# Routing of the first three batches spread over the attention heads, and the first expert's weights split inside the last heads

## What is computed

```python
q_n, k_n = rmsnorm(q, g_q), rmsnorm(k, g_k)
attn = softmax(q_n @ k_n.T / 8);  x = attn @ v          # 48 heads of 448 x 64
logits = (x / |x|) @ (emb / |emb|).T / tau               # x as 1792 rows of 768
expert = argmax(logits);  gate = softmax(logits)[expert]
y = gate * (relu(x @ w1[expert]) @ w2[expert])           # w1 768x1024, w2 1024x768
h = y @ w_in;  out = max(0.01 * h, h) @ w_out            # 768 -> 2048 -> 768
```

## Time and profile before

| | |
|---|---|
| time of the profiled execution, span | 1319.03 us, 1317.3 us |
| median of 3 runs | 1318.18 us |
| PE busy | 1237.8 us, 94% |
| DVE busy | 891.9 us, 68% |
| ACT busy | 748.0 us, 57% |
| POOL busy | 558.2 us, 42% |
| mean granted TensorE clock, share of full | 0.972 |
| attention / experts / feed-forward, about | 0 to 378, 378 to 802, 802 to 1317 us |

### The profile page before, as it was taken

One profiled execution on the slowest core, in us unless ns is written; L12 is line 12 of the kernel. 1 busy time (PEld: TensorE's weight loads), 2 busy tenths in 40 slices (PEclk: granted clock), 3 DMA queues, 4 the chain that ended last, 5 costly groups with the idle time before them and its releaser, 6 DMA issues. The chain is left out here.

```text
span 1317.3 us, 21043 instructions
## 1 busy us (share of the span) xinstructions
PE 1237.8 (94%) x6906; PEld 1101.8 (84%) x6906; DVE 891.9 (68%) x1267; ACT 748.0 (57%) x1420; POOL 558.2 (42%) x638
## 2 busy tenths in 40 slices
PE   5999999997878899999999986999999999999998
PEld 4888888876767789888999975899999999999997
DVE  4889999997574899999999993454432235552222
ACT  4999999996661688778888863222241122221111
POOL 6888888887632666656767660000000000000000
PEclk8999999999879999999999996999999999999999
DMA  1222222221711367655474114112132222211122
GB/s 50 58 71 70 67 70 71 71 65 45 240 32 36 131 240 261 250 204 198 166 260 143 59 37 133 36 48 73 56 101 56 89 66 75 76 43 49 54 85 71
DMA packets 101866, 131.94 MB, mean 100 GB/s; under 512 B 28664, under 2 KB 81144, under 8 KB 101760
## 3 DMA queue, kind: packets, MB, share of 16 engines
q1 hardware_dynamic: 94304, 108.58, 26.7%
q0 software_dynamic: 3360, 16.52, 3.5%
q10 hardware_dynamic: 4096, 5.51, 1.2%
HBM read 186.80 MB, written 19.27 MB: 156 GB/s over the span
## 5 line engine op out<-in xcount | busy, mean ns | idle before, releaser
L1057 ACT CAST w_hi<-w_raw 128x768 fp32r<-128x768 f32 (+1 forms) x280 | 238.8, 931 | 22.3 <-DMA w_raw<-moe_w_in 13.4
L1248 DVE TENSOR_TENSOR w_lo<-w_raw,w_hi 128x1024 fp32r<-128x1024 f32 x79 | 173.5, 2232 | 1.7 <-ACT w_hi L1057 1.6
L1665 DVE TENSOR_TENSOR out_lo<-out_raw,out_hi 128x384 fp32r<-128x384 f32 x64 | 35.7, 558 | 171.3 <-ACT out_hi L1574 171.3
L1456 PE MATMUL ps_acc<-yT_hi,in_hi 128*128 128x448 f32 x384 | 142.1, 370 | 2.1 <-DVE yT_lo L1651 2.1
L533 DVE TENSOR_TENSOR pT_lo<-ps_pt,pT_hi 112x448 fp32r<-112x448 f32 x192 | 115.1, 620 | 42.1 <-ACT pT_hi L474 41.9
L1486 PE MATMUL ps_acc<-gT_hi,out_hi 128*128 128x448 f32 x384 | 143.0, 372 | 0.0
L1457 PE MATMUL ps_acc<-yT_hi,in_lo 128*128 128x448 f32 x384 | 141.2, 368 | 0.0
L1458 PE MATMUL ps_acc<-yT_lo,in_hi 128*128 128x448 f32 x384 | 141.0, 367 | 0.0
L1488 PE MATMUL ps_acc<-gT_lo,out_hi 128*128 128x448 f32 x384 | 140.9, 367 | 0.0
L1487 PE MATMUL ps_acc<-gT_hi,out_lo 128*128 128x448 f32 x384 | 140.8, 367 | 0.0
L1568 ACT ACTIVATE small_h<-ps_acc 128x448 f32<-128x448 f32 x64 | 34.9, 546 | 181.2 <-PE ps_acc L1458 181.2
(11 more groups left out here) (226 smaller groups left out, 3042.0 us busy)
## 6 DMA issues: line engine op xcount, KB each, us to landing
w_raw<-moe_w_in SPq DMA_DIRECT2D x80, 1536.0 KB
in_raw<-moe_w_in_in SPq DMA_DIRECT2D x32, 384.0 KB, 3.3
out_raw<-moe_w_out_in SPq DMA_DIRECT2D x64, 192.0 KB, 2.4
qk_raw<-q_in SPq DMA_DIRECT2D x48, 112.0 KB, 2.0
qk_raw<-k_in SPq DMA_DIRECT2D x48, 112.0 KB, 2.1
v_raw<-v_in SPq DMA_DIRECT2D x48, 112.0 KB, 2.0
x_rows<-x_tok SPq DMA_DIRECT2D x48, 112.0 KB, 2.5
in_raw<-x_rows SPq DMA_DIRECT2D x16, 336.0 KB, 4.0
```

Source lines behind the costliest of these rows:

```text
L1057: act.copy(out[:, c, :], raw[:, c, :]).then_inc(s_hi, 1)
L1248: dve.tensor_tensor(w1_lo[:, c, :], w1_raw[:, c, :], w1_hi[:, c, :].bitcast(F32), ALU.subtract).then_inc(s_w1lo, 1)
L1456: pe.matmul(h, in_hi[u][:, c, :], yT_hi[:, c, cols], start=c == 0, stop=False)
```

## The change

1. Early routing is done batch by batch (b = 0, 1, 2). With head = (m-1) mod 12 in the rounds behind batch b, POOL does `choice(b, ...)` in rounds head = 1, 2, 4, 5, 6, 7, 8, in small instructions between `add_logits` and the next round's `split_k`; DVE keeps the reductions, and PE gets six small matmuls for each batch (`early_ranks(b)`, before two in all). The old chains on DVE in rounds 38 to 42, and the two POOL stretches of six `in_lane` each, are gone.
2. `s_pick` comes in POOL's round 43 (head = 6 of b = 2). SP loads w1 in step n = N - 3 = 45 and w2 in step 46, each one step earlier.
3. The gather of the first rows moves from POOL's round 45 to round 47, behind `lo_first(1)`, three small steps of `pick`, and `guard_sums(47)`.
4. The first w1 is split in the last heads: ACT casts chunk 0 at the end of round 46, 1 and 2 at the end of 47, 3 and 4 in round 48, 5 in 49; POOL does `w_lo` of 0 to 3 there, and of 4, 5 and three chunks of w2 at the start of `experts`. `product1(0)` is whole, in front of `place`.
5. `x_tok` holds one batch: DVE waits in `store_x` for the store of the head 12 before.
6. The late chain keeps one operand of each two-input step in PSUM, and finds blocks by comparing with a table of edges in place of integer shifts. `slot_in` is made once for all items; two one-element DVE instructions for each item are gone.

```diff
                     store(n - LAG)
-                if n == N - 2:
+                if n == N - 3:
                     sp.wait_ge(s_pick, 1)
                     e = sp.value_load(rt["item_expert"][0:1, 0:1], min_val=0, max_val=E - 1)
                     first_weights(e, w1, w1_raw, C1, s_w1_in)
-                if n == N - 1:
+                if n == N - 2:
                     first_weights(e, w2, w2_raw, C2, s_w2_in)
             for n in range(N - LAG, N):
                 store(n)
...
+            def choice(b, step):
+
+                js = slice(b * T, (b + 1) * T)
+                pool.wait_ge(s_route, STEPS * b + step)
+                if step == 1:
+                    for j in range(T):
+                        last = pool.tensor_scalar(is_top[:, j, :], logits[:, b * T + j, :], top[:, b * T + j:b * T + j + 1], None, ALU.is_equal)
+                    last.then_inc(s_route, 1)
+                if step == 2:
+                    pool.tensor_tensor(is_top[:, :, :], is_top[:, :, :], e_index[:, :, :], ALU.mult).then_inc(s_route, 1)
+                if step == 4:
+                    for j in range(T):
+                        last = pool.tensor_scalar(hot[:, b * T + j, :], e_index[:, j, :], first_top[:, b * T + j:b * T + j + 1], None, ALU.is_equal)
+                    last.then_inc(s_route, 1)
+                if step == 5:
+                    pool.wait_ge(s_ranks, b + 1)
+                    if b == 0:
+                        pool.tensor_copy(counts[:, b, :], added[:, :]).then_inc(s_route, 1)
+                    else:
+                        pool.tensor_tensor(ranks[:, :, :], ranks[:, :, :], counts[:, b - 1, :].unsqueeze(1).to_broadcast([R, T, E]), ALU.add)
+                        pool.tensor_tensor(counts[:, b, :], counts[:, b - 1, :], added[:, :], ALU.add).then_inc(s_route, 1)
+                if step == 6:
+                    pool.tensor_tensor(ranks[:, :, :], ranks[:, :, :], hot[:, js, :].bitcast(F32), ALU.mult).then_inc(s_route, 1)
+                if step == 8:
+                    for j in range(T):
+                        last = pool.tensor_scalar(beyond[:, j, :], rt["edges"][:, 1:], rank_f[:, j:j + 1], None, ALU.is_le)
+                    last.then_inc(s_route, 1)
+                if step == 10:
+                    pool.tensor_scalar(lane_f[:, :], blk_f[:, js], -float(P), None, ALU.mult).then_inc(s_route, 1)
+                if step == 11:
+                    pool.tensor_tensor(lane_f[:, :], lane_f[:, :], rank_f[:, :], ALU.add).then_inc(s_route, 1)
+                if step > 11:
+                    j = b * T + step - 12
+                    pool.tensor_scalar(in_lane[:, j, :], rt["lane_index"][:, :], lane_f[:, step - 12:step - 11], rt["row_plus"][:, j:j + 1],
+                                       ALU.is_equal, ALU.mult).then_inc(s_route, 1)
+
+            def pick(step):
+
+                pool.wait_ge(s_choose, step if step < 7 else step - 1)
...
+                    pool.tensor_tensor(most_e[:, :], most_e[:, :], e_index[:, 0, :], ALU.mult).then_inc(s_choose, 1)
+                if step == 4:
+                    pool.wait_ge(s_route, STEPS * (B - 2) + 11)
+                    pool.tensor_scalar(rt["item_expert"][:, 0:1], rt["chosen"][0:1, :], float(E), None, ALU.add).then_inc(s_pick, 1)
+                    pool.tensor_scalar(in_first_block[:, :], blk_f[:, 0:J0], 0.0, None, ALU.is_equal).then_inc(s_choose, 1)
+                if step == 5:
...
+            def gather_first():
+                pool.wait_ge(s_row_first, 1)
+                for h in range(H):
+                    pool.wait_ge(s_x_out[h], 16 * (B - 1))
+                pool.indirect_dma_start(out=x_first, out_offset=None, in_=x_rows[0:R * J0, :],
+                                        in_offset=bass.IndirectOffsetOnAxis(ap=row_first[:, 0:1], axis=0)).then_inc(s_x_first, 16)
+
+            def lo_first(c):
+                pool.wait_ge(s_w1hi, c + 1)
+                pool.tensor_tensor(w1_lo[:, c, :], w1_raw[:, c, :], w1_hi[:, c, :].bitcast(F32), ALU.subtract).then_inc(s_w1plo, 1)
...
+            def early_routing(m):
+
+                b, head = (m - 1) // H - 1, (m - 1) % H
+                if 0 <= b < B - 1:
+                    if head == 1:
+                        choice(b, 1)
+                        choice(b, 2)
+                    if head == 2:
+                        choice(b, 4)
+                    if head == 4:
+                        choice(b, 5)
+                        choice(b, 6)
+                    if head == 5:
+                        if b == B - 2:
+                            pick(1)
+                            pick(2)
+                        choice(b, 8)
+                    if head == 6:
+                        choice(b, 10)
+                        choice(b, 11)
+                        if b == B - 2:
+                            pick(4)
+                            pick(5)
+                    if head == 7:
+                        if b == B - 2:
+                            pick(6)
+                        choice(b, 12)
+                        choice(b, 13)
+                    if head == 8:
+                        choice(b, 14)
+                        choice(b, 15)
+                    if b == B - 2 and head == 10:
...
+                if m == N - 1:
+                    lo_first(1)
+                    for step in (7, 8, 9):
+                        pick(step)
...
+                early_routing(m)
+                if m == N - 2:
+                    lo_first(0)
+            lo_first(2)
             add_logits(N - 2)
+            lo_first(3)
...
+            def hi_first(c):
+                act.wait_ge(s_w1_in[2 * c // C1], 16)
+                act.copy(w1_hi[:, c, :], w1_raw[:, c, :]).then_inc(s_w1hi, 1)
+
             for m in range(-2, N + 2):
                 if 0 <= m - 1 < N:
...
+                if m == N - 2:
+                    hi_first(0)
+                if m == N - 1:
+                    hi_first(1)
+                    hi_first(2)
+                if m == N:
+                    x_hi_first()
+                    hi_first(3)
+                    hi_first(4)
+                if m == N + 1:
+                    hi_first(5)
 
...
+                if n >= H:
+                    dve.wait_ge(s_x_out[n % H], 16 * (n // H))
+                    dve.wait_ge(s_lg, n - H + 1)
                 dve.wait_ge(s_rs, n + 1)
-                dve.tensor_tensor(x_tok[:, :, bass.ds(n, 1), :].rearrange("p t o x -> p t (o x)"),
...
 
     def pool1(s):
-        return (0, 1, 2) if s == 0 else (1, 4)
+        return range(C1) if s == 0 else (1, 4)
 
     def pool2(s):
-        return (1, 4, 6) if s == 0 else (1, 5)
+        return (0, 1, 2) if s == 0 else (1, 5)
 
...
             def block_starts():
 
+                dve.tensor_tensor(ahead[:, :, :], rt["turned"][:, :].unsqueeze(2).to_broadcast([R, E, E]),
+                                  rt["turned"][:, :].unsqueeze(1).to_broadcast([R, E, E]), ALU.is_gt)
                 dve.wait_ge(s_tot, 1)
-                dve.tensor_reduce(totals[:, :], ps_tot.rearrange("p (j e) -> p e j", e=E), AX.X, ALU.add).then_inc(s_step, 1)
-                dve.wait_ge(s_step, 5)
-                dve.scalar_tensor_tensor(block_i[:, :], totals[:, :], float(P - 1), rt["counts"][:, :], ALU.add, ALU.add).then_inc(s_step, 1)
+                dve.tensor_reduce(totals, ps_tot.rearrange("p (j e) -> p e j", e=E), AX.X, ALU.add).then_inc(s_step, 1)
                 dve.wait_ge(s_step, 6)
-                dve.tensor_scalar(block_i[:, :], block_i[:, :], 7, None, ALU.logical_shift_right).then_inc(s_step, 1)
+                dve.tensor_tensor(count, totals, counts, ALU.add).then_inc(s_step, 1)
                 dve.wait_ge(s_step, 7)
-                dve.tensor_copy(blocks[:, :], block_i[:, :]).then_inc(s_step, 1)
+                dve.tensor_tensor(over[:, :, :], count.unsqueeze(2).to_broadcast([R, E, R * J // P]),
+                                  rt["edges"][:, :].unsqueeze(1).to_broadcast([R, E, R * J // P]), ALU.is_gt).then_inc(s_step, 1)
                 dve.wait_ge(s_step, 8)
-                dve.tensor_tensor(passed[:, :, :], rt["ahead"][:, :, :], blocks[:, :].unsqueeze(1).to_broadcast([R, E, E]), ALU.mult).then_inc(s_step, 1)
+                dve.tensor_reduce(p_blocks, over[:, :, :], AX.X, ALU.add).then_inc(s_step, 1)
                 dve.wait_ge(s_step, 9)
-                dve.tensor_reduce(start[:, :], passed[:, :, :], AX.X, ALU.add).then_inc(s_step, 1)
+                dve.tensor_tensor(passed[:, :, :], ahead[:, :, :], p_blocks.unsqueeze(1).to_broadcast([R, E, E]), ALU.mult).then_inc(s_step, 1)
+                dve.wait_ge(s_step, 10)
+                dve.tensor_reduce(start, passed[:, :, :], AX.X, ALU.add).then_inc(s_step, 1)
...
```

More of the change, by code:

```diff
@@ L32, in attention @@
     EARLY = H * (B - 1)
+    STEPS = 16
+    RANKED = [H * (b + 1) + 3 for b in range(B - 1)]
     DM = H * D
@@ L872, in load_x @@
```

(15 more changed lines are left out.)

407 lines of the change are left out of this document (177 added, 230 removed).

## The result

The changed kernel takes 1332.87 us, median of 4 runs (1330.51 to 1336.52); the kernel before, now with 4 runs, takes 1317.18. The ratio of the runs is 1.0135, 95% interval 1.0085 to 1.0186, while the two medians are 15.7 us apart, 1.2%. So it is slower by a little over 1%, near the 1336 of the forecast. Its profiled execution took 1330.51 us, with a span of 1328.5 against 1317.3: +11.2. That is less than the medians say, since the profiled execution of the changed kernel was the fastest of its four, and that of the kernel before (1319.03) above its median.

The account below looks back on a forecast made before the run. All engines were taken to wait in a circle, so 94% of POOL's inserted time reaches the end. Terms summed to +18.1 on 1319.0 profiled: 1337.1, or 1336 median (1330 to 1342 its own); whole range 1317 to 1349.

Parts of the forecast that it names:

- (1): Attention: the old early routing, with its gather and side effects, goes; -24.6 us.
- (2): Attention rounds: POOL's new small routing steps, 94% of their time on the path; +24.5 us.
- Rival (C): POOL's small pointer instructions in attention cost 0.55 us each, 8.5 us more in all, 1345; chance 0.12.
- (A): Rival: POOL absorbs its routing steps in its idle time in attention, 17 us less, 1320; chance 0.15.
- (3): Attention rounds: DVE's reductions and PE's six small matmuls for each batch; +1.5 us (0 to 4).
- (4): SP's queue: loads of head 46 wait behind w1, stalling ACT 10.9 us; +13.3 with the clock (0 to 20).
- Rival (B): The weights in SP's queue don't hold up the loads of the last heads, 1323; chance 0.15.
- (5): Last heads: ACT's casts of chunks 0 to 2 of the first weights; +2.5 us (1 to 4).
- (6): End of attention: PE waits 6.0 us for the later gather; +7.4 with loss of clock (4 to 10).
- (7): Start of the experts: `product2(0)` ends 32 us behind it, before 38.5; -6.5 us (-2 to -11).
- Rival (D): Start of the experts: POOL holds DVE and the chain waits behind `product1(0)`, gain only -2, 1341; chance 0.06.
- (8): Item loop's two one-element instructions for each item, and the output ring's waits: nothing counted for either.

Follow-up runs that it names:

- e4_lanes: Changed kernel with the eight `in_lane` of batches 0 and 1 moved, one in a round, in front of `invert_rms`; 1327.64 us, ratio 1.0090 to the kernel before.
- e7_spread: Changed kernel with the eight `in_lane` of batches 0 and 1 one in a round, left at the round's end; 1331.40 us, ratio 1.0134 to before.
- e1_loads: Changed kernel with w1 and w2 both issued in SP's last step, behind the loads of head 47; 1322.83 us, ratio 1.0058 to the kernel before.
- e8_casts: Changed kernel with weights behind loads, gather early, POOL's routing in front of `invert_rms`, and ACT's casts of chunks 1 and 2 in round 48; 1294.27 us.
- e9_split: Kernel before with POOL subtracting chunks 0, 1, 2 of the first w2 in place of 1, 4, 6; timed once, 1310.4 us.
- e6_once: Kernel before with all items' slots made once and two one-element DVE instructions in each item gone; 1308.51 us, ratio 0.9950.
- e3_slots: Changed kernel with two one-element DVE instructions put back in each item; 1334.52 us, ratio 1.0148 to the kernel before.
- e11_tables: e8_casts with POOL's constant tables of rounds 4 to 7 moved in front of the next `invert_rms`; 1292.15 us, ratio 0.9813 to the kernel before.

## Why the prediction was right

The sum, +18.1 profiled, gave 1336; measured 1332.9 as a median, a profiled +11.2. The sign and most of the terms held. Against the sum the experts start 4.4 too late, and then 0.8, 7.2 and 3.3 come back that it did not have, at the start of the experts, in the item loop and behind it. That errors of both signs were in it, and that the medians lie 15.7 apart where the profiled executions lie 11.2, brought the forecast nearer to the median than its terms deserve: that part is luck.

**(1) and (2), POOL's steps one for one.** Right in size: predicted 8.2 us for a batch (with the reductions), measured 8.5 and 8.6. The small pointer instruction takes 0.31, and `in_lane` 0.85 at a pitch of two (timeline of after, POOL):

```profile
153.61 0.25 POOL L266 TENSOR_TENSOR logits<-logits,x_tok 112x32 f32<-112x32 f32 x1
153.84 1.24 POOL L293 TENSOR_SCALAR early_beyond<-edges,rank_f 112x13 f32<-112x13 f32 x4
155.03 0.73 POOL L222 TENSOR_TENSOR k_hl<-k_n,k_hl 112x256 fp32r<-112x256 f32 x1
```

Rival (C), 0.55 each, falls, and with it the fixed price of 0.5 that the prediction had estimated: 13 elements took 0.31 in all. (The rate used there is for two tensor inputs, and `in_lane` has one.) (A) falls for the place in which the steps stood. But the ground that the prediction gave, that all engines wait in a circle, was too general. The circle passes through `split_k`; POOL's free 0.66 stands in another place of its queue and was open to anyone who put work there (e4_lanes against e7_spread). The prediction looked at how much POOL was idle and not at where.

**(3)** The reductions and small matmuls do not show by themselves in the periods, and no run takes them out. What they cost of the 1.5 stays open.

**(4) Loads behind the weights.** Right in mechanism and near in size: wait 11.9 for 10.9, and 11.8 at the start of the experts for 13.3 with the clock. Head 47 cost next to nothing, as said. The prediction had both parts in its sum, the wait for `s_pick` and the transfer; e1_loads takes both away and cannot tell their shares. Rival (B) falls by it.

**(5) Casts.** 0.9 to 2.0 by e8_casts, for 2.5; up to 1.1 of the 2.0 is a difference in the granted clock one head earlier.

**(6) The gather, mis-sized.** The wait was 6.47 for 6.0. The loss of clock behind it was put at 1.4, "as less work is left". PE's 8.1 us of busy time from the transposes on all ran at 0.50, where the same work took 4.4 before, at 1.00 and 0.92. The difference, 3.7, goes with the clock. Last exponential to experts: +10.5 for the predicted 7.4. That is 3.1 of the 4.4 by which the experts start late; the other 1.3 was not taken apart.

**(7) The start of the experts.** -7.3 for -6.5, both holds at `late_cand` and `ahead` where they were predicted, each a little shorter. Rival (D) falls. The causes of the -7.3 were not separated. The changed kernel also has e9_split's other choice of chunks of w2, which the prediction did not price, and that alone made this stretch 3.7 shorter in the kernel before.

**(8) Counted as nothing, and that was wrong.** The item loop gave back 7.2. The prediction read DVE's slack in attention and did not look at DVE in the loop, where the windows have it busy for 20.00 of 20 us and the trace of before has four waits of PE for it. e6_once shows that these two alone were worth 5.6 us there. But they are not the whole cause in the changed kernel: put back into it (e3_slots) they bring no long item, so another entry to the loop, as in e9_split, which the prediction did not consider, is enough there too.

With (8) at -7.2 the sum would have been 1329.9 profiled, and with (6) at +10.5 as well 1333.0; the profiled execution took 1330.5. What is left is the 3.3 behind the loop and smaller pieces of both signs.

## What to carry over

Where several engines run in step, ask for each engine not only how long it is idle in a round but at which instruction, and put added work directly in front of that one: 0.80 us cost 0.14 there and 0.77 three instructions earlier in the queue. Issue large loads behind the small ones that somebody wants soon. If large loads cost nothing today because a stall hides them, expect to pay for them when that stall is taken away. Before an instruction is counted as nothing, look at its engine in the stretch where it stands. And when a step that gives a signal is moved, ask who waits for the signal.

## What was not expected

- The granted clock fell to 0.50 in the last heads of e11_tables while PE was fully busy, at a place where in e8_casts, the same program from round 8 on, it stayed at 1.00. In the two heads this execution took 3.2 us longer. What set it off was not found. A change in the last heads is better read by its waits than by its total.
- SP's issues themselves became slow behind the weights: the two of w2 took 4.45 us and the next q 1.99, where a usual q takes 0.3 to 0.4. Head 47, whose loads stood there, made ACT wait 0.81 us all the same.
- The stall behind the weights grew from 11.9 to 14.9 us when POOL's routing steps were moved, though neither the weights nor the loads were touched: the signal that the weights wait for had moved with them.
